# Chunked linear attention into a mixture of experts: the state's swap by DMA instead of a matmul, and another order at the passage

## What is computed

```python
for t in range(S):                       # q, k, v, a: (2, 8, 768, 48)
    new_re = ar * S_re - ai * S_im       # a is scaled to a magnitude below 0.999 first
    new_im = ar * S_im + ai * S_re
    S_re, S_im = (new_re + kv, new_im)   # kv = k[t] outer v[t]
    y[:, :, t] = einsum('bhd,bhde->bhe', q[:, :, t], S_re)
x = y as 1536 rows of 384
expert = argmax(x @ w_gate)              # softmax weight of it is kept
out[i] = gate * (relu(x[i] @ w1[expert]) @ w2[expert])    # the first 384 rows of an expert
out = ((out @ w_a) * (out @ w_b)) @ w_out
```

## Time and profile before

| | |
|---|---|
| time, median of 3 runs | 595.55 us (592.36 to 595.8) |
| profiled execution | 595.63 us, of which span 594.4 us |
| PE busy | 549.8 us, 92% of the span |
| DVE busy | 376.1 us, 63% |
| ACT busy | 266.8 us, 45% |
| POOL busy | 51.8 us, 9% |
| mean granted PE clock | 0.975 |

### The profile page before, as it was taken

The page is one execution under the profiler, slowest core; times in us unless marked ns, Lnnn a source line. Parts: engine busy times, 40 slices in busy tenths (PEclk is TensorE's granted clock), DMA queues, the critical chain, the costliest instruction groups (busy, mean ns, idle before and its releaser), DMA issues.

```text
span 594.4 us, 10223 instructions
## 1 busy us (share of the span) xinstructions
PE 549.8 (92%) x3800; PEld 487.9 (82%) x3801; DVE 376.1 (63%) x937; ACT 266.8 (45%) x565; POOL 51.8 (9%) x66
## 2 busy tenths in 40 slices
PE   0499687889999999999999999999999999999996
PEld 0277354779999998999999998888888888888886
DVE  5899999968888878888898886444412212122121
ACT  5666557732222136777778783433331122322112
POOL 1000000001121116000000000350020000200002
PEclk9977799999999999999999999999999999999999
DMA  8999032498222124876666629830010000100001
GB/s 321 273 387 322 1 150 73 176 221 251 80 61 71 42 71 157 303 238 206 206 237 204 207 103 161 145 95 0 1 53 1 1 0 1 53 1 0 1 0 54
DMA packets 46321, 73.28 MB, mean 123 GB/s; under 512 B 16520, under 2 KB 38792, under 8 KB 45384
## 3 DMA queue, kind: packets, MB, share of 16 engines
q1 hardware_dynamic: 44360, 67.97, 37.2%
q0 software_dynamic: 1920, 4.75, 2.5%
HBM read 55.76 MB, written 16.97 MB: 122 GB/s over the span
## 4 chain that ended last, share of the span: by engine, by line
PE 75%; DVE 15%; ACT 5%; DMA 3%; issue 1%; POOL 0%; DVEq 0%; SPq 0%; POOLq 0%; ACTq 0%
PE psum L1323 25%; PE psum L1296 12%; PE psum L1129 10%; PE psum L1092 9%; PE psum L848 4%; DVE region L372 3%; PE psum L695 3%; PE psum L822 3%; PE psum L850 2%; DVE region L377 2%; PE psum L867 2%; ACT region L465 2%; DMA xrow<-sorted_x 2%; DVE region L421 1%; PE psum L280 1%
## 5 line engine op out<-in xcount | busy, mean ns | idle before, releaser
L1338 DVE TENSOR_TENSOR ga<-ga,psum 128x512 f32<-128x512 f32 x36 | 24.8, 688 | 129.7 <-PE psum L1323 122.5
L1342 ACT ACTIVATE gh<-ga 128x512 fp32r<-128x512 f32 x36 | 22.8, 632 | 80.7 <-DVE ga L1338 78.4
L1336 ACT ACTIVATE ga<-psum 128x512 f32<-128x512 f32 x36 | 21.5, 598 | 76.2 <-PE psum L1323 76.2
L1129 PE MATMUL psum<-hh,w2h 128*128 128x224 f32 x192 | 53.7, 279 | 0.0
L1092 PE MATMUL psum<-xh,w1h 128*128 128x224 f32 x192 | 53.0, 276 | 0.5 <-DVE xl L963 0.5
L280 PE MATMUL psum<-region,ident 128*128 128x384 f32 (+1 forms) x42 | 24.6, 677 | 30.9 <-ACT region L290 22.7
L1129 PE MATMUL psum<-hh,w2l 128*128 128x224 f32 x192 | 52.7, 274 | 0.0
L1092 PE MATMUL psum<-xh,w1l 128*128 128x224 f32 x192 | 52.7, 274 | 0.0
L1092 PE MATMUL psum<-xl,w1h 128*128 128x224 f32 x192 | 52.7, 274 | 0.0
L1129 PE MATMUL psum<-hl,w2h 128*128 128x224 f32 x192 | 52.6, 274 | 0.0
L1296 PE MATMUL psum<-woh,gh 128*128 128x384 f32 x144 | 48.3, 335 | 0.4 <-DVE gl L1344 0.4
(11 more groups left out here) (198 smaller groups left out, 1463.5 us busy)
## 6 DMA issues: line engine op xcount, KB each, us to landing
raw<-w SPq DMA_DIRECT2D x14, 1536.0 KB
sorted_x<-region SPq DMA_DIRECT2D x8, 579.0 KB, 13.9
queries<-qk SPq DMA_DIRECT2D x4, 1152.0 KB, 25.8
xrow<-sorted_x SPq DMA_DIRECT2D x7, 579.0 KB, 6.8
region<-x_rows SPq DMA_DIRECT2D x14, 288.0 KB
queries<-w SPq DMA_DIRECT2D x2, 1536.0 KB
x_rows<-region SPq DMA_DIRECT2D x5, 576.0 KB, 3.1
region<-a SPq DMA_DIRECT2D x2, 1152.0 KB, 9.4
```

Of the source, the lines that this page charges most:

```text
L1129: m = nc.tensor.matmul(bank[YB0 + c][:, 0:cols], wx[:, f, c * P:(c + 1) * P], xx[:, f, 0:cols], start=f == 0 and i == 0, stop=f == NF - 1 ...
L1336: m = act.done(ss.activation(ga[f % 2][:], ba[:, 0:TT], ACT.Copy))
L1338: m = dve.done(tt(ga[f % 2][:], ga[f % 2][:], bb[:, 0:TT], ALU.mult))
L1342: m = act.done(ss.activation(gh[f % GB3][:], ga[f % 2][:], ACT.Copy))
```

## The change

The matrix swap is gone. The sum goes into zs[n % 2], and two DMAs on SP's queue copy its lower 48 partitions into the upper ones of zx[n % 2] and the other way round. The sign is moved into Wi: the fourth row of `ends` is written by ACT in two halves, one with scale -1. The product with Wr becomes four activations per unit that write PSUM; two DVE operations make Z of both, one unit later than before in the order. `masked` comes right behind the sum. V of batch 1 and the weights of expert 0 are loaded in 19 parts on GpSimd's queue, one in each of units 1 to 19. At the passage placing, ranks and choice of chunks 13 and 14 stand elsewhere, counting comes behind the ranks, `turn_first` goes by tile and not by column, late products of chunk 14 come before those of 15, and the first two blocks of `hidden(0)` go by column.

```diff
-            dve.done(vv.tensor_copy(ends[:, 2:4, :].rearrange("p i (r d) -> p i r d", r=2),
-                                    walk(AT_Z[1] + lo_at + D, [SA, 2], [0, 2], [1, D])))
+            dve.done(vv.tensor_copy(ends[:, 2, :].rearrange("p (r d) -> p r d", r=2),
+                                    walk(AT_Z[1] + lo_at + D, [0, 2], [1, D])))
+            act.wait(*m_step[HALF - 1])
+            act.done(ss.activation(ends[:, 3, 0:D], flat(AT_Z[2] + lo_at + D, D), ACT.Copy))
+            m_minus = act.done(ss.activation(ends[:, 3, D:C2], flat(AT_Z[2] + lo_at + D, D), ACT.Copy, scale=-1.0))
...
-            pe.wait(m_ends, *free[b])
+            pe.wait(m_ends, m_minus, *free[b])
...
+            zr = [bank[i][0:C2, 0:YB * DE] for i in (7, 1)]
...
+                return dve.done(vv.tensor_reduce(out=X[:, t, DM:DM + 1], in_=ex[:, t, :], axis=AXX, op=ALU.add))
+
+            def place_chunk(t):
+
+                if t < LATE - 1:
+                    m_den = counted(t)
+                dve.wait(m_lx[t], m_rk[t])
                 m_tk[t] = dve.done(tt(sel[:, t, :], rk[0:L], ohb[:, t, :], ALU.mult))
                 dve.wait(m_tk[t])
                 m = dve.done(vv.tensor_reduce(out=rank[:, t:t + 1], in_=sel[:, t, :], axis=AXX, op=ALU.add))
+                if t >= LATE - 1:
+                    m_den = counted(t)
...
-            sp.dma_start(flat(AT_KQ, P // 2 * D, L), v[1]).then_inc(s_v[1], 16)
-            sp.wait_ge(s_vw[1], 16)
-            sp.dma_start(flat(AT_VW[1], VWN, L), vw_rows[1]).then_inc(s_vwin[1], 16)
+            VP = 4
+            VCUT = P // 2 * D // VP
+            parts = [(flat(AT_KQ + i * VCUT, VCUT, L), v[1][:, i * VCUT:(i + 1) * VCUT], s_v[1]) for i in range(VP)]
+            parts.append((flat(AT_VW[1], VWN, L), vw_rows[1], s_vwin[1]))
+            WP = 2 * KC
+            cuts = [(c, slice(h * F // 2, (h + 1) * F // 2)) for c in range(KC) for h in range(2)]
+            parts += [(y1[:, c, cut], x1[:, c, cut], s_w0) for i, (c, cut) in enumerate(cuts)]
+            parts += [(y2[:, f, :], x2_[:, f, :], s_w0) for f in range(NF)]
...
+                r = n % 2
                 if j:
                     dve.wait(z_done[gr])
-                    m = dve.done(tt(zm[0], Z[gr], bank[6][0:C2, 0:YB * DE], ALU.add))
+                    m = dve.done(tt(zs[r], Z[gr], bank[6][0:C2, 0:YB * DE], ALU.add))
...
                 m_add[n] = m
+                sp.wait_ge(dve.sem, m[1])
+                for i in range(2):
+                    sp.dma_start(zx[r][i * D:(i + 1) * D, :], zs[r][(1 - i) * D:(2 - i) * D, :]).then_inc(s_ex[r], 16)
+                n_ex[r] += 32
...
+            def turned_by_real(n):
+
+                act.wait(m_add[n], m_ends)
+                for i, p in enumerate(heads(n)):
+                    cut = slice(i * DE, (i + 1) * DE)
+                    m_zr[n] = act.done(ss.activation(zr[n % 2][:, cut], zs[n % 2][:, cut], ACT.Copy, scale=Wr[:, p:p + 1]))
+
             def turned_state(n):
 
-                pe.wait(m_add[n])
-                if m_turned_z:
-                    pe.wait(m_turned_z)
-                return pe.done(nc.tensor.matmul(bank[7][0:C2, 0:YB * DE], swap[:], zm[0], start=True, stop=True))
+                j, gr = units[n]
+                r = n % 2
+                w = Wi[:, gr * YB * NC + j:(gr + 1) * YB * NC:NC].unsqueeze(2).broadcast_to([C2, YB, DE])
+                dve.wait(m_ends)
+                vv.wait_ge(s_ex[r], n_ex[r])
+                m = dve.done(tt(heads_of(zx[r]), heads_of(zx[r]), w, ALU.mult))
+                dve.wait(m, m_zr[n], m_y[n])
+                z_done[gr] = dve.done(tt(Z[gr], zr[r], zx[r], ALU.add))
 
             for n in range(NUNIT):
...
-                if n % GB == 0 and n:
+                if n % GB == 0 and n and done < LATE:
                     choose(done)
...
-                if n == GB:
-                    for s_, x, y in ((s_w1, w1[0].rearrange("(c p) f -> p c f", p=P), raw_0[0]),
-                                     (s_w2, w2[0].rearrange("(f p) n -> p f n", p=P), raw_0[1])):
-                        sp.dma_start(y.rearrange("p (c f) -> p c f", f=x.shape[-1]), x).then_inc(s_, 16)
+                if 1 <= n <= len(parts):
+                    if n == 1:
+                        pool.wait(m_prod[3, "q", 0], m_turn[-1], m_kx[3])
+                        g.wait_ge(s_vw[1], 16)
+                    y, x, s_ = parts[n - 1]
+                    g.dma_start(y, x).then_inc(s_, 16)
                 if more and n:
                     state_in(n)
+                if n and n + 1 < NUNIT and n != LATE * GB:
+                    masked(n + 1)
+                if n > 1 and units[n - 1][0] < NC - 1:
+                    turned_state(n - 1)
...
-                    dve.wait(m_add[n], m_ends)
-                    m_zr = dve.done(tt(z3[1], z3[0], wv(Wr), ALU.mult))
+                    turned_by_real(n)
+                if n == 1:
+                    turned_state(0)
                 if n:
-                    if n + 1 < NUNIT:
-                        masked(n + 1)
                     queried(n)
-                if n % GB == 0 and done >= LATE - 1:
+                if n == (LATE + 1) * GB:
+                    choose(LATE)
+                if n == LATE * GB:
                     ranks(done)
                     place_chunk(done)
...
+                    masked(n + 1)
+                if n == LATE * GB + 1:
+                    sp.wait_ge(pe.sem, m_y[NUNIT // 2 - 1][1])
+                    sp.wait_ge(s_sc, 16 * LATE)
+                    sp.dma_start(rows_0, sorted_x[0, 0:CAP, :].rearrange("(i p) c -> p i c", p=P)).then_inc(s_row0, 16)
+            ranks(LATE)
+            place_chunk(LATE)
             choose(TAU - 1)
...
             turn_first(2)
+            add_late(LATE, 0)
             pe.wait(m_tk[TAU - 1], m_so[TAU - 1])
             m_tl = pe.done(nc.tensor.matmul(rk, onesb[:], so[:, TAU - 1, :], start=True, stop=True))
+            for c in range(1, KC):
+                add_late(LATE, c)
             for c in range(KC):
-                add_late(LATE, c)
                 add_late(TAU - 1, c)
...
+                for c in range(KC if at_first else 0):
+                    for f in range(2):
+                        pe.wait(m_1[0][f], m_x[c])
+                        m = w1_mm(cols, f, c)
```

More of the change, by code:

```diff
@@ L138, in build @@
         m_ones = pool.done(g.memset(onesb[:], 1.0))
-        m = pool.done(g.memset(swap[:], 0.0))
-        pool.wait(m)
+        pool.wait(m_ones)
         c_id = pool.done(g.affine_select(out=ident[:], in_=ident[:], compare_op=ALU.not_equal, fill=1.0, base=0,
@@ L145, in build @@
                                           pattern=[[1, L]], channel_multiplier=-1))
[L147 to L151, removed]
         HALF = L // 2
@@ L646, in build @@
             pe.wait(*last)
+            act.wait(*(free[7] or ()))
             dve.wait(m_set, m_mask)
@@ L985, in build @@
             dve.wait(*z_done)
-            nc.scalar.wait_ge(s_w1, 16)
+            nc.scalar.wait_ge(s_w0, 16 * (WP + NF))
             m_w1, m_x0 = [], []
+            dve.done(vv.memset(one8, 1.0))
+            dve.wait(m_tl)
+            D_(vv.tensor_scalar(kept, rk, float(CAP), None, ALU.min))
+            D_(vv.tensor_tensor_scan(out=cumk, data0=one8, data1=kept, initial=0.0, op0=ALU.mult, op1=ALU.add))
+            D_(tt(fst, cumk, kept, ALU.subtract))
+            dve.done(vv.tensor_copy(first[:], fst))
+            m_first = dve.done(vv.tensor_copy(nkept[:], kept))
             for f in range(NF):
@@ L990, in build @@
                 if f == 2:
-                    dve.done(vv.memset(one8, 1.0))
-                    dve.wait(m_tl)
-                    D_(vv.tensor_scalar(kept, rk, float(CAP), None, ALU.min))
-                    D_(vv.tensor_tensor_scan(out=cumk, data0=one8, data1=kept, initial=0.0, op0=ALU.mult, op1=ALU.add))
-                    D_(tt(fst, cumk, kept, ALU.subtract))
-                    dve.done(vv.tensor_copy(first[:], fst))
-                    m_first = dve.done(vv.tensor_copy(nkept[:], kept))
                     for c in range(KC):
@@ L1076, in hidden, with w1_mm @@
             m_1 = w1_marks
+            def w1_mm(cols, f, c):
+                for i, (wx, xx) in enumerate(((w1h, xh), (w1h, xl), (w1l, xh))):
+                    m = nc.tensor.matmul(bank[HB0 + f % 4][:, 0:cols], wx[:, c, f * P:(f + 1) * P], xx[:, c, 0:cols],
+                                         start=c == 0 and i == 0, stop=c == KC - 1 and i == 2)
+                    if wide and cols <= (XT_N - 1) * P and f == 0 and c == 0 and i == 0:
+                        assert pe.done(m) == m_t2
+                return m
             def mm(cols):
@@ L1082, in mm @@
                     pe.wait(m_x2)
-                for f in range(NF):
-                    b = HB0 + f % 4
+                for c in range(KC if at_first else 0):
+                    for f in range(2):
+                        pe.wait(m_1[0][f], m_x[c])
```

(4 more changed lines are left out.)

67 lines of the change are left out of this document (28 added, 39 removed).

## The result

The changed kernel is **slower: 615.0 us** (median of 4 executions, 612.49 to 651.17) against 595.67 before (4 executions, 592.36 to 596.27); the ratio is 1.032 (1.026 to 1.038). The profiled execution is the slowest of the four, 651.17 us with a span of 649.9 us; the ratio is taken from the other three, and the profile shows what they have in a smaller dose.

A forecast was written before the change was run, and what follows sets the result against it. PE was taken to bound the recurrence, by about 0.5 us over DVE. Swap -10.9, loaded exchanges +1.0, end factors +1.0 and passage -0.9 gave -9.8 us, from 595.55 to 585.8 us; range 582.3 to 592.5.

The forecast's parts named there:

- Where the wait stands: Recurrence: exchange waits stay hidden up to 2.7 us in quiet chunks; 2.8 us under loads costs +1.0 us.
- rival 3: Passage: the longer PE wait keeps the clock at 1.2 GHz over the late products; 590 us, chance 0.10.
- The swap leaves PE: Recurrence: 26 swaps of 0.42 us come off PE, -10.9 us; a full chunk takes 5.53 us.
- DVE, ACT and mask ahead: Recurrence: Wr product moved to ACT, about 0.2 us per activation, and earlier mask cost nothing; DVE stays under PE.
- The exchange's L: Recurrence: time from sum to exchanged state, 2.2 to 2.5 us when quiet, 2.8 taken under loads.
- Weights and V in parts … Nothing: Recurrence: 19 part loads on GpSimd's queue cost nothing, as nobody waits for scatters before the passage.
- rival 1: Recurrence: exchanges later than allowed in all chunks, about 3.1 us; 590.2 us, chance 0.20.
- Rival 2: Recurrence: exchanges take 4 us in 13 chunks, making the kernel slower; 602.6 us, chance 0.06.
- End factors: Ahead of the recurrence: copies moved to ACT delay PE's transposes and the turns; +1.0 us, bounds +0.2 to +1.2.
- Passage: Recurrence to expert stage: reordering removes a 0.51 us wait and some more; -0.9 us, bounds -1.5 to 0.
- Sum of the quiet terms: Whole kernel: swap, loaded exchanges, end factors and passage together; -9.8 us.

The follow-up runs named there:

- e3: Kernel before, with PE waiting once, in unit 2, for six GpSimd memsets; 633.19 us.
- e2: Changed kernel without the exchange DMAs, the turned state made from the sum itself; 587.9 us, ratio 0.985.
- e12: e9 with the 19 parts issued one per unit, up to unit 19, instead of two; 595.48 us, ratio 0.999.
- e1: Changed kernel again without any edit, on another chip; 626.09 us, ratio 1.042.
- e4: Changed kernel plus one dummy 96x224 product on PE ahead of the wait for Z in each unit with a state; 612.75 us.
- e5: Changed kernel without the 14 weight loads, V's five parts one per unit from unit 5 behind the exchange; 608.92 us, ratio 1.022.
- e6: Changed kernel with all 19 parts, each held until its own unit's state products are done; 612.52 us, ratio 1.026.
- e7: Changed kernel plus three dummy 128x384 products ahead of the wait for Z in units 2, 3, 18 and 19; 617.4 us, ratio 1.035.
- e11: e3 plus four dummy 128x384 products on PE one unit later; 603.53 us, ratio 1.010 against the kernel before.
- e9: Changed kernel with PE's matrix swap kept in units 0 to 11, exchanges in units 12 to 29, all parts issued by unit 10; 589.22 us, ratio 0.987.
- e10: e9 with every unit swapping on PE, so all of the change but the exchange; 594.96 us, ratio 0.997.
- e8: Kernel before, with PE waiting once, in unit 2, for two GpSimd memsets; 595.7 us, ratio 0.999.

## Why the prediction was wrong

**The step that failed** is "Where the wait stands", and with it rival 3. I priced a wait of PE at its own length ("the price per chunk is L + 2.85 - 6.37"), asked for the clock only in the passage, and so left it out of the sum for the recurrence. What decides is what PE's wait does to the clock of a stretch that hardly brings it back: one wait of 2.35 us cost 37 us in the median (e3). The forecast was 585.8; with the clock taken out the profiles of the changed kernel come to some 589 and 587, and without exchanges it measured 587.9. For the three executions of 612.5, 614.1 and 615.9 us only the mean clocks are there: 0.951, 0.940 and 0.938 against 0.979 in an e2 of 587.0. At two levels, 1.2 and 2.4 GHz, an estimate is twice the difference in mean clock times the span: 35, 49 and 52 us more at half clock, so 17, 23 and 24 us lost. They lie 27, 28 and 30 us over the forecast, so most of it is clock; the other 10, 5 and 6 are worked out and not shown in a profile of these executions, but waits for late exchanges at full clock, about 4 us over six units in e12, are of that size. At half clock these hide, as PE takes nearly twice as long for what lies beside them. The row that I set against rival 3, a wait of 1.27 us at 110.36 without a fall, stands ahead of transposes of 128 columns in a row, and single waits of 2.29 and 2.01 us in the recurrence passed too; one row couldn't exclude it. All waits of PE of 0.9 us and more that the profiles show in the recurrence at full clock, with what the clock did after them:

| | waits, us |
|---|---|
| clock fell to 0.50 | 2.48 and 1.40 (after), 1.64 (e1), 2.35 (e3), 1.18 (e4), 2.34 (e5), 1.76 (e6), 2.40 (e7), 2.35 (e11) |
| it held | 2.29 (e1), 1.59 and 1.09 (e5), 2.01, 1.40 and 1.32 (e6), 1.47 and 0.97 (e4), 0.94 (e12) |

**The swap leaves PE**: right in kind, a tenth too large. A full chunk takes 5.61 us in e9 and in e2, forecast 5.53, so a swap is worth (6.37 - 5.61)/2 = 0.38 us and not the 0.42 between two starts, and 26 of them 9.9 us, not 10.9. 16 units that count for 14 (28 and 29 lie at the passage) were forecast at 5.9 us; e9 against e10 measured 5.7, but 4.6 to 5.4 at like clock. That 5.7 lies so near 5.9 is in part luck.

**DVE, ACT and mask ahead**: right. An activation with Wr takes 291 ns in the median rather than 0.2 us; e9's ACT is far from full, and no wait of PE leads to it.

**The exchange's L**: 2.0 us to landing in the median against 1.8, and a second issue of 0.5 to 0.6, as estimated; DVE waits 0.41 us at most for it in e9's quiet chunks. The prediction's 2.1 us, an estimate from the Trainium skill, page "DMA: Bandwidth & Descriptors", section "Anatomy of one DMA", rests on a figure given there for DMAs issued by GpSimd; these are issued by SP, and here the trace decides. Under the loads I took L = 2.8 with a bound of 3.1. The longest landing alone is 4.3 us, and DVE waits up to 3.5. Forecast +1.0 over nine chunks; e12 shows about 4 us over three, so this term was mis-sized several times over even before the clock.

**"Weights and V in parts … Nothing"**: wrong. I looked at who waits for the parts and for POOL, and not at what the parts delay. I did name the shared engines as a rule behind rival 1 and gave it 0.20; its premise was true (e5, e6, e12), its result of 590.2 wasn't, since it lacked the clock. Rival 2 had the right side by a mechanism that didn't set the time: it wanted a late exchange in all 13 full chunks, and in e9 and e12 it is late only while parts come in.

**End factors**: right. In absolute times the turns start only 0.16 us later (110.52 against 110.36), but the two profiles don't have ACT at the same place by then. Counted from the start of ACT's last full-width step ahead of them (L410 before, L403 after) they start 1.15 us later before and 2.32 us later after:

```profile
109.21 0.52 ACT L410 ACTIVATE region<-region 128x384 f32<-128x384 f32 x1
```

```profile
108.20 0.52 ACT L403 ACTIVATE region<-region 128x384 f32<-128x384 f32 x1
```

All four profiles with the first stage of before have 1.15, all ten with that of the changed kernel 2.32 to 2.33. So this term measured +1.2 us, forecast +1.0 with a bound of +1.2.

**Passage**: PE waits 1.01 to 1.25 us ahead of turn_first (e9, e2; forecast 1 to 2), and the wait of 0.51 us ahead of the hidden products is gone. Forecast -0.9, and with end factors +0.1; e10 gives -1.3 to -2.0 for both, mask and order together, but +0.8 at like clock, where executions of one kernel differ by about that much. The sign is open, the size is small as forecast.

**Sum of the quiet terms**: -9.8 forecast; e2 gives 0.985 of 595.7, -8.8, with a new wait of 2.15 us that I hadn't looked for. At like clock it is less: e2 took 589.11 and 588.83 us at 0.972 and 0.975, where before on the same chip took 595.74 to 596.66 and 595.1, so 6.3 to 7.6 us.

## What to carry to other kernels

Before a wait is put into a stretch of short matmuls, ask what it does to the granted clock there, and whether anything in that stretch would bring the clock back; if not, the price is that what is left of the stretch takes nearly twice as long (1.9 times here), not the wait. A DMA on which the next step depends is sized with what all queues have in flight at that time, not by its bytes. An exchange by DMA is worth its place where it is quiet: cut the change by units, as e9 does. And when two kernels differ by 1%, compare executions of like mean clock before you credit the edit.

## What was not expected of the hardware

- A PE that is busy in 130.00 of 130 us stays at 0.50 (e1), while four long products bring the clock back within 5 us (e11). In six of seven profiles it also came back at the middle of the recurrence, where PE had run a few microseconds without products of 56 columns.
- One wait of 2.35 us costs 37 us in the median (e3), and waits of 1.2 to 2.5 us in the recurrence make the clock fall in some cases and not in others; 0.89 us never did, in ten executions (e8). Ahead of turn_first the clock fell around waits of 0.63 us (before), 0.90 (e10), 1.08 (e5), 1.10 (e12) and 1.17 (e7) and held over 0.57 (e8), 0.68 (e3), 0.93 (e6), 0.95 (e11), 1.01 (e9), 1.04 (e4) and 1.25 (e2). So length alone doesn't decide, and what does stays open.
- A copy of 42 KB within the core's memory lands 1.8 us after issue at best, 2.0 in the median and 4.3 in a kernel that loads 192 to 288 KB at a time on another engine's queue (after).
